# Reordering the head of the scan on ScalarE, VectorE and TensorE in a fused attention and expert kernel

## The chip, the cores and the metric

One core of a Trainium2 chip runs the whole program. The metric is the device time of one execution in microseconds (us). Three executions of the kernel before took 952.8, 953.1 and 955.27 us, median 953.1 us. Engines: PE is TensorE, DVE is VectorE, ACT is ScalarE, POOL is GpSimd, SP is SyncE, which issues most DMAs.

## What is computed

Three stages follow each other on 3072 tokens of width 384:

```python
# 1. delta rule attention, 32 heads of width 48, 768 steps
y[t] = q[t] @ state
state = state + beta[t] * outer(k[t], v[t] - k[t] @ state)      # k normalized
# 2. MLP 384 -> 2048 -> 384
h = x @ w_in;  g = maximum(0.01 * h, h);  x = g @ w_out
# 3. gated experts: argmax over 8 experts, two products 384 -> 1024 -> 384 for live tokens
y = gate_w * (maximum(x @ w1[e], 0) @ w2[e]);  out = x + y
```

## The kernel before, in words

The 768 steps are cut into G = 12 groups of 64. A group's recurrence is solved in closed form. It needs a product of k with the old state (z), the inverse of a small triangular system for each head (t, read as tT) applied to z (u), a correction (z2, u2), the output (y) and the new state (s). Each is done in two halves, r = 0 and r = 1. All matrices are fp16 pairs: a high half that ACT writes (a copy) and a low half, the rest after the high one, that DVE or POOL writes. Each product is three matmuls, high by high, low by high, high by low. So a scan step is a chain of PE product, DVE sum into fp32, ACT high half, DVE low half, next PE product.

The work is written out by hand as turns g with 16 steps f each; every engine has its own `turn` with the order of its steps. In a turn PE also runs the MLP: `up(g, f)` (L659 and on, first product, nine matmuls) and `down(g, f)` (L673 and on, second product, six matmuls), one of each in each step, shifted against the scan by 10 and 12 steps: in step f = 0 of turn g, `up` works on tile 6 of group g-1. Between them ACT does `hidden` (L937) and `hidden_high`, DVE `leaky` (L1294) and POOL `hidden_low` (L1604).

Other pieces that the change touches or that its steps meet:
- The head of the scan: PE `scan_z(g, r)` in f = 0, `scan_u(g, r)` in f = 1 (both L606, with s or z on the left). DVE `scan_z` (L1245) adds v to z, ACT `scan_z` writes its high half, DVE `scan_z_low` (L1250) its low half. `scan_u(g, 0)` on PE waits for that low half and for `t_loaded`.
- The inverse of group g+1 is made on DVE in 31 links (`inverse`, L1210 link 0, L1213 link 1, a wide product of 128x512, L1216 link 2, then pairs L1224 and L1230). `SHARE` says how many links a step takes, one half of them (rounded up) ahead of `leaky` and the rest behind. Links of group g+2 begin in f = 15. Link 0 waits for `seed`, an ACT copy of 128x1024 in f = 14. The finished inverse takes `inverse_high` (ACT, f = 12) and `inverse_low` (DVE, L1237, f = 12). Then SP writes it to DRAM with two DMAs (L443) and, when they have landed, reads it back with eight (L453): the landing of these is `t_loaded`.
- `q_low(g+2, x)` on DVE: low half of q, 64x768, in f = 13 and 15; the transposes of q by SP wait for it in the next turn.
- Rows and scores: ACT `rows_out(g-1)` in f = 11 copies the MLP's two accumulators b_acc (after `down` tile 15) to x2. `down` of the next group starts in them in f = 12. `gate_x` transposes x2 on PE, `gate_s` makes the scores on PE in f = 14 (w = 0) and f = 15 (w = 1), and DVE `gate_s` (L1303) copies them to `logit`. PE's second scores wait for DVE's first copy (same bank b_gr).
- `p_high(g+1, st)` on ACT in f = 11 to 14: high half of the masked q k products that DVE (L1186) has written.

L826 is the helper line of all ACT copies, L1157 that of DVE's low halves by `lo`.

Of the kernel before, what the change touches and what calls it, by code (L numbers as in the profile page):

```python
# [19 lines left out]
def build(nc, q, k, v, beta, w_in, w_out, w_skip, w_gate, w1, w2, out):  # L20
# [18 lines left out]
    TT = 2  # L39
# [19 lines left out]
    with ctx:  # L59
# [272 lines left out]
        def up_at(g, f):  # L332
            n = g if f >= 10 else g - 1
            return (n, (f - 10) % FT) if is_group(n) else None
# [19 lines left out]
        LINKS = 3 + 2 * (HR - 1)  # L354


        SHARE = (1, 1, 4, 0, 4, 2, 3, 1, 4, 3, 5, 4, 0, 0, 0, 1)

        SECOND = (2, 2, 2, 2, 3, 3, 2, 0, 0, 0, 6, 6, 5, 0, 0, 0)
        SOON = 14  # L360
# [206 lines left out]
        def _(pe):  # L567
# [104 lines left out]

            def down(g, f):  # L673
                pe.wait_ge(g_lo, FT * g + f + 1)
                if f == 0 and g:
                    pe.wait_ge(x2_ready, TT * g)
                elif f == 0:
                    pe.wait_ge(w_ready, DT + 4)
                for w in range(TT):
                    for a, b in PARTS:  # L680
                        mm = pe.matmul(b_acc[w][:, 0:DM], g16[:, f % 4, a, w * P:(w + 1) * P],  # L681
                                       wt[1][:, b, f * DM:(f + 1) * DM],
                                       start=(f == 0 and (a, b) == PARTS[0]),
                                       stop=(f == FT - 1 and (a, b) == PARTS[2]))
                mm.then_inc(acc_done, 1)
# [138 lines left out]
        def _(act):  # L824
# [80 lines left out]
            def scan_u(g, r):  # L905
                act.wait_ge(u_done, 2 * g + r + 1)
                copy(u16[:, HI, pair(r)], b_ch[r][:, 0:WR]).then_inc(u_hi, 1)
# [25 lines left out]
            def hidden(g, f):  # L933
                act.wait_ge(h_done, FT * g + f + 1)
                if FT * g + f >= 2:
                    act.wait_ge(g_ready, FT * g + f - 1)
                act.activation(r32[:, f % 2, :], b_h[f % 2][:, 0:GT], ACT.Relu, scale=0.99).then_inc(h_relu, 1)  # L937
# [7 lines left out]
            def rows_out(g):  # L945
                act.wait_ge(acc_done, FT * g + FT)
                if g:
                    act.wait_ge(x2_stored, 64 * g)
                    act.wait_ge(tr_done, tr_at["g", g - 1, TT - 1])
                for w in range(TT):  # L950
                    copy(x2[:, w, :], b_acc[w][:, 0:DM], 1.0 / (H_S * WO_S)).then_inc(x2_ready, 1)
# [38 lines left out]
            def turn(g):  # L990
                scan, nxt, ahead = is_group(g), is_group(g + 1), is_group(g + 2)
                gate, third = is_group(g - 1), is_group(g + 3)
                for f in range(FT):
                    if scan and f in (1, 3, 4, 6):
                        {1: scan_z, 3: scan_z2, 4: scan_u2, 6: scan_s}[f](g, 1)
                    if scan and f == 5:
                        scan_y(g, 1)
                    if gate and f in (13, 14):
                        gate_x(g - 1, f - 13)
                    if scan and f in (8, 9):  # L1000
                        x_high(g, f - 8)
                    if ahead and 7 <= f < 11:
                        gram_out(g + 2, f - 7)
                    if nxt and 11 <= f < 15:
                        p_high(g + 1, f - 11)
                    if nxt and f == (12 if g else 13):
                        inverse_high(g + 1)
                    if up_at(g, f):
                        hidden(*up_at(g, f))
                    if scan and f == 1:  # L1010
                        scan_u(g, 0)
                    if up_at(g, f):
                        hidden_high(*up_at(g, f))
                    if scan and f in (0, 2, 3, 4, 5):
                        {0: scan_z, 2: scan_z2, 3: scan_u2, 4: scan_y, 5: scan_s}[f](g, 0)
                    if g == G and f == 10:
                        act.wait_ge(h_done, FT * G)
                        split_hi(0, 0, 0)
                    if gate and f == 11:
                        rows_out(g - 1)  # L1020
                    if scan and f == 1:
                        scan_u(g, 1)
                    if nxt and f == 3:
                        a21_high(g + 1)
                    if g == 0 and f in (0, 1):
                        kn_high(2, f)
                    if third and f == k_part(g, "squares"):
                        squares(g + 3)
                    if third and f == k_part(g, "root"):
                        root(g + 3)  # L1030
                    if third and f - k_part(g, "split") in (0, 1):
                        kn_high(g + 3, f - k_part(g, "split"))
                    if ahead and f in (12, 13):
                        q_high(g + 2, f - 12)
                    if ahead and f == 14:
                        seed(g + 2)
                    if (g, f) in ((G - 1, 8), (G, 3)):
                        exponents(g - G + 1)
# [109 lines left out]
        def _(dve):  # L1148
# [174 lines left out]
            def turn(g):  # L1323
                scan, nxt, ahead = is_group(g), is_group(g + 1), is_group(g + 2)
                gate, third = is_group(g - 1), is_group(g + 3)
                sums = {0: scan_z, 2: scan_z2, 3: scan_u2, 5: scan_s}
                lows = {0: scan_z_low, 1: scan_u_low, 2: scan_z2_low, 3: scan_u2_low}
                for f in range(FT):
                    n, inv = (g + 2, ahead) if f >= SOON else (g + 1, nxt)
                    share = SECOND if n == 1 else SHARE  # L1330
                    at = sum(share[SOON:f]) if f >= SOON else sum(share[SOON:]) + sum(share[:f])
                    mid, end = at + (share[f] + 1) // 2, at + share[f]
                    if scan and f - 1 in sums:
                        sums[f - 1](g, 1)
                    if f == 0 and is_group(g - 2):
                        gate_s(g - 2, 1)
                    if f == 15 and gate:
                        gate_s(g - 1, 0)
                    if nxt and 11 <= f < 15:
                        gram_p(g + 1, f - 11)  # L1340
                    if inv and mid > at:
                        inverse(n, at, mid)
                    if gate and f in (13, 14):
                        gate_x_low(g - 1, f - 13)
                    if scan and f - 1 in lows:
                        lows[f - 1](g, 1)
                    if scan and f in (8, 9):
                        x_low(g, f - 8)
                    if up_at(g, f):
                        leaky(*up_at(g, f))  # L1350
                    if scan and f in sums:
                        sums[f](g, 0)
                    if inv and end > mid:
                        inverse(n, mid, end)
                    if scan and f in lows:
                        lows[f](g, 0)
                    if ahead and f in (13, 15):
                        q_low(g + 2, (f - 13) // 2)
                    if nxt and f == 4:
                        a21_low(g + 1)  # L1360
                    if nxt and f == (12 if g else 13):
                        inverse_low(g + 1)
                    if third and f == k_part(g, "sum"):
                        norm_sum(g + 3)
                    if third and f == k_part(g, "norm"):
                        norm(g + 3)
                    if g == G and f == 10:
                        split_lo(0, 0, 0)
                    if (g, f) in ((G - 1, 6), (G, 1)):
                        route_best(g - G + 1)  # L1370
                    if (g, f) in ((G - 1, 7), (G, 2)):
                        route_hot(g - G + 1)
                    if (g, f) in ((G - 1, 11), (G, 6)):
                        route_prob(g - G + 1)
                        route_rank(g - G + 1)
                    if g == G - 1 and f >= 12:
                        seats(2 * (f - 12), 2 * (f - 11))
                    if g == G and f < 9:
                        seats(2 * f + 8, min(2 * f + 10, NT - TT))
                    if g == 0 and f in (3, 4):  # L1380
                        split_w_out(f - 1)
                    if g == 0 and f in (4, 5):
                        q_low(1, f - 4)
# [372 lines left out]
```

## Time and profile before

| what | value |
|---|---|
| median of three executions | 953.1 us |
| the profiled execution | 950.53 us, its span 948.8 us |
| PE busy | 805.5 us, 85% |
| DVE busy | 644.0 us, 68% |
| ACT busy | 502.7 us, 53% |
| POOL busy | 412.1 us, 43% |
| mean granted PE clock | 0.944 |

The span begins with 130 us of loading and of a first, thinly filled turn. The turns run to about 705 us, the routing ends at about 720 us, and the experts take the rest. In the timeline a row has the start and the length in us, the engine, line and operation, what is written from what, and in brackets how long the engine had been idle before it and what ended that.

### The profile page before, as it was taken

What the parts mean: (1) busy time and instruction counts of PE and PEld (TensorE: products, weight loads), DVE (VectorE), ACT (ScalarE), POOL (GpSimd) and SP (SyncE); (2) the same over time, 40 slices, a digit from 0 to 9 for tenths busy, and PEclk for the clock granted to TensorE, in tenths of its full rate; (3) what the DMA queues carried; (4) which work ended last, traced back from release to release, by engine and by line L of the source; (5) the groups of instructions that cost most, each with busy time, mean ns of one, the idle gap of its engine ahead of it and who ended that gap; (6) DMA issues with size and microseconds to landing.
All of it is one profiled execution on the core that took longest, in us unless ns stands there. A gap on an engine that the chain in (4) does not pass through costs nothing.

```text
span 948.8 us, 27901 instructions
## 1 busy us (share of the span) xinstructions
PE 805.5 (85%) x10858; PEld 650.3 (69%) x10859; DVE 644.0 (68%) x1303; ACT 502.7 (53%) x1099; POOL 412.1 (43%) x500
## 2 busy tenths in 40 slices
PE   0314869899999999998989999999984899999986
PEld 0214648787777778787868777778753687788864
DVE  5478868787877778787877787765566835523372
ACT  4436546667575766566665657454453624322161
POOL 4404334536262635344453624253223655644463
PEclk9856699999999999999999999999995999999998
DMA  8774654575667766647656465332363943611100
GB/s 240 128 217 64 121 106 89 109 112 103 121 120 111 132 108 126 122 88 128 111 114 114 87 110 110 68 66 56 86 249 105 321 174 104 228 66 45 38 24 16
DMA packets 309830, 109.97 MB, mean 116 GB/s; under 512 B 284930, under 2 KB 301364, under 8 KB 309344
## 3 DMA queue, kind: packets, MB, share of 16 engines
q1 hardware_dynamic: 304000, 94.63, 48.0%
q0 software_dynamic: 3232, 7.64, 2.3%
q10 hardware_dynamic: 2496, 6.29, 1.8%
q8 instruction: 69, 1.13, 0.5%
q14 instruction: 33, 0.27, 0.1%
HBM read 60.39 MB, written 20.46 MB: 85 GB/s over the span
## 4 chain that ended last, share of the span: by engine, by line
PE 37%; DVE 24%; ACT 14%; issue 13%; DMA 6%; SPq 3%; POOL 2%; DVEq 1%; ACTq 0%; POOLq 0%
PE b_acc L807 8%; PE b_acc L681 8%; PE b_h L791 7%; PE b_h L668 7%; DVE stage L1294 5%; PE b_ch L606 4%; ACT ga L826 3%; ACT stage L937 3%; DVE inv L1230 2%; DVE inv L1224 2%; ACT stage L826 2%; ACT operands L826 2%; DMA natq<-x_dram,id_in 2%; ACT z L826 2%; DVE inv L1213 1%
## 5 line engine op out<-in xcount | busy, mean ns | idle before, releaser
L1604 POOL TENSOR_TENSOR stage<-stage 128x256 f16<-128x256 f32 x192 | 138.3, 720 | 289.5 <-ACT stage L826 288.6
L681 PE MATMUL b_acc<-wt,stage 128*128 128x384 f16 x1152 | 222.7, 331 | 6.2 <-ACT stage L826 5.7
L668 PE MATMUL b_h<-stage,wt 128*128 128x256 f16 x1728 | 221.7, 274 | 4.4 <-DVE stage L1294 3.2
L668 PEld LDWEIGHTS b_h<-stage,wt 128*128 128x128 f16 x1728 | 159.8, 98 | 24.6 <-DVE stage L1294 4.5
L681 PEld LDWEIGHTS b_acc<-wt,stage 128*128 128x128 f16 x1152 | 107.5, 98 | 63.2 <-POOL stage L1604 8.8
L826 ACT ACTIVATE stage<-stage 128x256 f16<-128x256 f32 x192 | 80.0, 417 | 125.5 <-DVE stage L1294 125.5
L1294 DVE SCALAR_TENSOR_TENSOR stage<-b_h,stage 128x256 f32<-128x256 f32 x192 | 80.9, 421 | 72.4 <-ACT stage L937 72.1
L807 PE MATMUL b_acc<-wt,operands 128*128 128x384 f16 x576 | 101.6, 327 | 6.0 <-DVE operands L1522 6.0
L791 PEld LDWEIGHTS b_h<-y,wt 128*128 128x128 f16 x1728 | 100.6, 100 | 8.3 <-issue 6.4
L791 PE MATMUL b_h<-y,wt 128*128 128x128 f16 x1728 | 103.3, 223 | 3.2 <-DVE y L1157 2.8
L572 PE MATMUL b_gr<-operands 128*128 128x128 f16 x576 | 45.1, 235 | 52.3 <-DMA operands<-operands 21.1
L1230 DVE TENSOR_REDUCE inv<-inv 128x30 f32<-128x90 f32 (+4 forms) x180 | 84.8, 471 | 5.6
L1594 POOL TENSOR_TENSOR operands<-masked,operands 128x512 f16<-128x512 f32 x48 | 57.2, 1193 | 70.1 <-ACT operands L826 70.0
L937 ACT ACTIVATE stage<-b_h 128x256 f32<-128x256 f32 x192 | 72.1, 375 | 22.5 <-PE b_h L668 22.5
L807 PEld LDWEIGHTS b_acc<-wt,operands 128*128 128x128 f16 x576 | 54.6, 98 | 39.5 <-DVE operands L1522 8.3
L572 PEld LDWEIGHTS b_gr<-operands 128*128 128x128 f16 x576 | 40.0, 106 | 57.0 <-issue 48.2
L1110 ACT ACTIVATE operands<-b_h 128x512 f16<-128x512 f32 x48 | 28.5, 594 | 85.1 <-PE b_h L791 85.1
L1224 DVE TENSOR_TENSOR inv<-a_sys,inv 128x60 f32<-128x60 f32 (+4 forms) x180 | 70.0, 389 | 1.8
L606 PE MATMUL b_ch<-z,operands 128*128 128x48 f16 x1152 | 40.2, 189 | 31.1 <-DVE z L1250 24.5
L606 PEld LDWEIGHTS b_ch<-z,operands 128*128 128x128 f16 x1152 | 38.1, 100 | 38.9 <-issue 29.7
L1522 DVE SCALAR_TENSOR_TENSOR operands<-b_h,operands 128x512 f16<-128x512 f32 x48 | 33.0, 688 | 46.1 <-ACT operands L1110 46.0
L1157 DVE SCALAR_TENSOR_TENSOR wt<-operands,wt 128x1536 f16<-128x1536 f32 x32 | 57.5, 1805 | 7.3 <-ACT wt L826 5.9
(174 smaller groups left out, 1300.9 us busy)
## 6 DMA issues: line engine op xcount, KB each, us to landing
operands<-in_moe_w_dram SPq DMA_DIRECT2D x16, 1536.0 KB, 7.0
a_sys<-a_dram SPq DMA_DIRECT2D x24, 256.0 KB, 4.2
natq<-in_q_dram SPq DMA_DIRECT2D x24, 192.0 KB, 4.0
raw_v<-in_v_dram SPq DMA_DIRECT2D x24, 192.0 KB, 3.7
stage<-y SPq DMA_DIRECT2D x96, 48.0 KB, 2.1
x_dram<-stage SPq DMA_DIRECT2D x24, 192.0 KB, 2.9
out_dram<-stage SPq DMA_DIRECT2D x24, 192.0 KB, 3.0
natk<-in_k_dram SPq DMA_DIRECT2D x22, 192.0 KB, 3.9
```

The lines of the kernel that those rows point to most:

```text
L572: mm = pe.matmul(b_gram[st % 2][:, p * P:(p + 1) * P], kT[g % 2][:, a, u, :], rhs[:, b, u, :], start=(p == 0 and (a, b) == PARTS[0]), stop ...
L606: mm = pe.matmul(b_ch[r][:, i * D:(i + 1) * D], lhs[:, a, u, :], rhs[:, b, u * D:(u + 1) * D], start=(first and i == 0 and (a, b) == PARTS ...
L668: mm = pe.matmul(b_h[f % 2][:, 0:GT], wt[0][:, a, d * FF + f * P:d * FF + (f + 1) * P], xT[:, g % 2, b, d, :], start=(i == 0), stop=(i == ...
L681: mm = pe.matmul(b_acc[w][:, 0:DM], g16[:, f % 4, a, w * P:(w + 1) * P], wt[1][:, b, f * DM:(f + 1) * DM], start=(f == 0 and (a, b) == PAR ...
L791: mm = pe.matmul(b_h[half][:, f * P:(f + 1) * P], wt[i][:, a, d * F1 + fc:d * F1 + fc + P], xgT[:, b, d * P:(d + 1) * P], start=(f == 0 an ...
L807: mm = pe.matmul(b_acc[0][:, 0:DM], e16[:, half, a, f * P:(f + 1) * P], wt[i][:, b, w0:w0 + DM], start=(half == 0 and f == 0 and (a, b) == ...
L826: return act.activation(o, i, ACT.Copy, scale=scale)
L937: act.activation(r32[:, f % 2, :], b_h[f % 2][:, 0:GT], ACT.Relu, scale=0.99).then_inc(h_relu, 1)
L1224: dve.tensor_tensor(inv[:, 1:3].rearrange("p k (r i) -> p k r i", i=BLK)[:, :, 0:rows, c:BLK], a[:, c - 2:c, c:BLK].unsqueeze(2).to_broadc ...
L1230: dve.tensor_reduce(t_next[:, 0:rows, c:BLK], planes.rearrange("p k (r i) -> p r i k", i=BLK)[:, 0:rows, c:BLK], AX.X, ALU.add).then_inc(t ...
L1294: dve.scalar_tensor_tensor(g32[:, f % 4, :], b_h[f % 2][:, 0:GT], 0.01, r32[:, f % 2, :], ALU.mult, ALU.add).then_inc(g_ready, 1)
L1604: pool.tensor_tensor(g16[:, f % 4, LO, :], g32[:, f % 4, :], g16[:, f % 4, HI, :], ALU.subtract).then_inc(g_lo, 1)
```

## The change

In `SHARE` (groups 2 and on) one link of the inverse moves from step 0 to step 1: link 1, the wide product, now stands in f = 1 ahead of `leaky`, and link 2 behind it. On DVE, `scan_z(g, 0)` moves to the front of step 0, ahead of the inverse and `leaky`; `q_low(g+2, 1)` moves to the front of step 15; the copy of the first scores moves from the front of step 15 to step 14. On ACT, `scan_z(g, 0)` moves between `hidden` and `hidden_high` of step 0; in step 11 `p_high(g+1, 0)` and `rows_out(g-1)` move between `hidden` and `hidden_high`. On PE, `down(g, 0)` waits for the two copies of x2 one at a time, each ahead of the matmuls that overwrite its accumulator. No instruction is added or removed.

```diff
--- before.py
+++ after.py
@@ -354,7 +354,7 @@
         LINKS = 3 + 2 * (HR - 1)
 
 
-        SHARE = (1, 1, 4, 0, 4, 2, 3, 1, 4, 3, 5, 4, 0, 0, 0, 1)
+        SHARE = (0, 2, 4, 0, 4, 2, 3, 1, 4, 3, 5, 4, 0, 0, 0, 1)
 
         SECOND = (2, 2, 2, 2, 3, 3, 2, 0, 0, 0, 6, 6, 5, 0, 0, 0)
         SOON = 14
@@ -672,11 +672,11 @@
 
             def down(g, f):
                 pe.wait_ge(g_lo, FT * g + f + 1)
-                if f == 0 and g:
-                    pe.wait_ge(x2_ready, TT * g)
-                elif f == 0:
+                if f == 0 and not g:
                     pe.wait_ge(w_ready, DT + 4)
                 for w in range(TT):
+                    if f == 0 and g:
+                        pe.wait_ge(x2_ready, TT * (g - 1) + w + 1)
                     for a, b in PARTS:
                         mm = pe.matmul(b_acc[w][:, 0:DM], g16[:, f % 4, a, w * P:(w + 1) * P],
                                        wt[1][:, b, f * DM:(f + 1) * DM],
@@ -1001,23 +1001,27 @@
                         x_high(g, f - 8)
                     if ahead and 7 <= f < 11:
                         gram_out(g + 2, f - 7)
-                    if nxt and 11 <= f < 15:
+                    if nxt and 12 <= f < 15:
                         p_high(g + 1, f - 11)
                     if nxt and f == (12 if g else 13):
                         inverse_high(g + 1)
                     if up_at(g, f):
                         hidden(*up_at(g, f))
+                    if nxt and f == 11:
+                        p_high(g + 1, 0)
+                    if scan and f == 0:
+                        scan_z(g, 0)
                     if scan and f == 1:
                         scan_u(g, 0)
+                    if gate and f == 11:
+                        rows_out(g - 1)
                     if up_at(g, f):
                         hidden_high(*up_at(g, f))
-                    if scan and f in (0, 2, 3, 4, 5):
-                        {0: scan_z, 2: scan_z2, 3: scan_u2, 4: scan_y, 5: scan_s}[f](g, 0)
+                    if scan and f in (2, 3, 4, 5):
+                        {2: scan_z2, 3: scan_u2, 4: scan_y, 5: scan_s}[f](g, 0)
                     if g == G and f == 10:
                         act.wait_ge(h_done, FT * G)
                         split_hi(0, 0, 0)
-                    if gate and f == 11:
-                        rows_out(g - 1)
                     if scan and f == 1:
                         scan_u(g, 1)
                     if nxt and f == 3:
@@ -1334,10 +1338,14 @@
                         sums[f - 1](g, 1)
                     if f == 0 and is_group(g - 2):
                         gate_s(g - 2, 1)
-                    if f == 15 and gate:
-                        gate_s(g - 1, 0)
+                    if ahead and f == 15:
+                        q_low(g + 2, 1)
+                    if scan and f == 0:
+                        scan_z(g, 0)
                     if nxt and 11 <= f < 15:
                         gram_p(g + 1, f - 11)
+                    if f == 14 and gate:
+                        gate_s(g - 1, 0)
                     if inv and mid > at:
                         inverse(n, at, mid)
                     if gate and f in (13, 14):
@@ -1348,14 +1356,14 @@
                         x_low(g, f - 8)
                     if up_at(g, f):
                         leaky(*up_at(g, f))
-                    if scan and f in sums:
+                    if scan and f in sums and f:
                         sums[f](g, 0)
                     if inv and end > mid:
                         inverse(n, mid, end)
                     if scan and f in lows:
                         lows[f](g, 0)
-                    if ahead and f in (13, 15):
-                        q_low(g + 2, (f - 13) // 2)
+                    if ahead and f == 13:
+                        q_low(g + 2, 0)
                     if nxt and f == 4:
                         a21_low(g + 1)
                     if nxt and f == (12 if g else 13):
```

## Rows read from the trace of the kernel before

**Rows 1.** The page: PE's granted clock in 40 slices, tenths of full speed

```profile
PEclk9856699999999999999999999999995999999998
```

**Rows 2.** Waits of PE over the span: us in total, times, longest

```profile
PE b_ch L606 <- DVE z L1250: 24.5, 11, 5.1
...
PE b_ch L606 <- DMA operands<-t_dram: 4.4, 2, 4.1
...
PE b_gr L708 <- DVE logit L1303: 2.0, 9, 0.2
```

**Rows 3.** Timeline of PE at the heads of turns 5 and 6

```profile
341.96 0.76 PE L606 MATMUL b_ch<-z,operands 128*128 128x48 f16 x24 [1.97 <-DVE z L1250]
...
387.19 0.77 PE L606 MATMUL b_ch<-s,operands 128*128 128x48 f16 x24
...
389.38 1.14 PE L668 MATMUL b_h<-stage,wt 128*128 128x256 f16 x9
392.48 0.71 PE L606 MATMUL b_ch<-z,operands 128*128 128x48 f16 x19 [1.96 <-DVE z L1250]
```

**Rows 4.** Timeline of DVE and ACT from turn 5's step 13 to turn 6's step 1

```profile
382.11 1.41 DVE L1157 SCALAR_TENSOR_TENSOR nq<-natq,nq 64x768 f16<-64x768 f32 x1
...
387.26 0.28 DVE L1210 SCALAR_TENSOR_TENSOR inv<-a_sys,inv 128x32 f32<-128x32 f32 x1 [1.42 <-issue]
387.47 0.42 DVE L1294 SCALAR_TENSOR_TENSOR stage<-b_h,stage 128x256 f32<-128x256 f32 x1
...
387.92 0.95 DVE L1157 SCALAR_TENSOR_TENSOR nq<-natq,nq 64x768 f16<-64x768 f32 x1
...
389.11 1.29 DVE L1213 TENSOR_TENSOR inv<-a_sys 128x512 f32<-128x512 f32 x1
...
390.65 0.54 DVE L1245 SCALAR_TENSOR_TENSOR scan<-raw_v,b_ch 128x384 f32<-128x384 f32 x1
...
391.22 0.52 ACT L826 ACTIVATE z<-scan 128x384 f16<-128x384 f32 x1
...
391.78 0.56 DVE L1250 TENSOR_TENSOR z<-scan,z 128x384 f16<-128x384 f32 x1 [0.59 <-ACT z L826]
...
392.73 0.68 DVE L1216 TENSOR_TENSOR a_sys<-a_sys,inv 128x512 f32<-128x512 f32 x1
```

**Rows 5.** Timeline: the inverse's low half in turns 5 and 6, SP's transfers of it

```profile
379.30 0.75 DVE L1237 TENSOR_TENSOR inv<-inv 128x256 f16<-128x256 f32 x2
...
431.29 0.75 DVE L1237 TENSOR_TENSOR inv<-inv 128x256 f16<-128x256 f32 x2
...
380.08 1.63 SPq L443 DMA_DIRECT2D t_dram<-inv  x2
383.48 5.32 SPq L453 DMA_DIRECT2D operands<-t_dram  x8
```

**Rows 6.** Timeline: the same low half and PE's product after it, turns 1 and 11

```profile
125.44 1.22 DVE L1237 TENSOR_TENSOR inv<-inv 128x256 f16<-128x256 f32 x2
...
137.13 0.58 PE L606 MATMUL b_ch<-z,operands 128*128 128x48 f16 x10 [4.10 <-DMA operands<-t_dram]
...
631.81 0.75 DVE L1237 TENSOR_TENSOR inv<-inv 128x256 f16<-128x256 f32 x2
...
643.54 0.78 PE L606 MATMUL b_ch<-z,operands 128*128 128x48 f16 x24 [0.31 <-DMA operands<-t_dram]
```

**Rows 7.** Timeline of turn 5, steps 11 and 12: rows, masked products, first down

```profile
376.20 0.85 ACT L826 ACTIVATE stage<-b_acc 128x384 f32<-128x384 f32 x2
...
377.38 0.63 ACT L826 ACTIVATE operands<-masked 128x512 f16<-128x512 f32 x1 [0.32 <-DVE masked L1186]
...
377.20 1.14 PE L681 MATMUL b_acc<-wt,stage 128*128 128x384 f16 x6 [0.69 <-ACT stage L826]
```

**Rows 8.** Windows at the head of turn 6: busy by engine, PE clock, DMA share

```profile
389.60:392.80 3.20, 1.24 (x22) 0.93 (x20) 2.61 (x6) 0.94 (x2) 0.67 (x1) 1.00 0.69 159
393.00:396.20 3.20, 3.20 (x41) 2.19 (x39) 2.14 (x6) 1.43 (x4) 0.67 (x1) 0.50 0.89 198
```

## The prediction

> **What bounds the kernel now.** I read the page first: PE is busy 85% of the span (table above), and its clock is full in nearly every slice from the sixth on [rows 1]. So a turn is set by PE's own work plus what PE waits for. The waits of PE name that: 24.5 us in 11 waits for the low half of z, 4.4 us for the inverse's transfer, 2.0 us for the copy of the first scores [rows 2]. The timeline shows where the first sits. In turn 6 PE starts `up` at 389.38, ends it at 390.52, and starts `scan_u(6,0)` only at 392.48 [rows 3]. The turn before had its own `scan_u(5,0)` at 341.96, so a turn takes 392.48 - 341.96 = 50.5 us.
>
> Why z is late stands on DVE [rows 4]. Link 0 waits 1.42 us; what releases it is the seed, a copy by ACT. Then come `leaky`, the second half of q (0.95), the scores copy, the wide product (1.29), `leaky` again (0.34 us to the start of the sum), and only at 390.65 the sum of z, though PE's z product had ended at 387.19 + 0.77 = 387.96 [rows 3]. After the sum come the ACT copy (0.52) and the low half, ended at 391.78 + 0.56 = 392.34.
>
> The second thing that `scan_u(g,0)` waits for is the inverse. Its low half ends at 379.30 + 0.75 = 380.05, SP issues two DMAs, then from 383.48 eight more, 5.32 us of issue [rows 5]. How long this trip takes to landing, two other heads tell, where PE did wait for it: 137.13 - (125.44 + 1.22) = 10.47 us in turn 1 and 643.54 - (631.81 + 0.75) = 10.98 us in turn 11 [rows 6]; mean 10.7. So in turn 6 it lands at about 380.05 + 10.7 = 390.8, and `scan_u` at 12.43 us after the low half is 1.7 us later than the inverse allows.
>
> **The clock.** In the window 389.6 to 392.8, where PE is busy 1.24 of 3.2 us, the granted clock is 1.00 (2.4 GHz); in the window behind it, 0.50 (1.2 GHz), with PE busy throughout [rows 8]. Heads 4, 8 and 10 have the same pair of windows, four falls in all. Its price: from `scan_u` to the inverse's next low half the turn after head 5 takes 380.05 - 341.96 = 38.09 us, the turn after head 6 takes 431.29 + 0.75 - 392.48 = 39.56 us [rows 3, 5], so 1.47 us a drop.
>
> **The change, part by part.**
>
> 1. Second half of q to the front of step 15. It now runs inside the 1.42 us in which DVE waits for the seed. It takes 0.95, or 1.41 as the first half does beside a POOL instruction [rows 4]; either end fits. Gain on DVE's chain ahead of z: 0.95. SP waits for it only in the next turn. Cost nothing, cover the seed.
>
> 2. Sum of z ahead of the inverse and `leaky`. With the wide product gone from step 0 too, DVE goes from link 0 (387.26) to `leaky` (0.21 later), 0.34 later to the scores copy, about 0.2 later to the sum: 388.0 on the old clock. The sum to the end of the low half took 392.34 - 390.65 = 1.69 [rows 4]. z would be ready at 389.7, 2.6 us earlier. `leaky(g-1,6)` moves behind the sum by 0.54, but DVE then waits 0.59 for ACT's z copy anyway, and this fills with it. `hidden_high` moves behind ACT's z copy (0.52); its `down` is a step and a half away.
>
> 3. The wide product in step 1. It stands between z's second sum and its second low half, where link 2 (half as long) stood. On my clock: sum 389.7 to 390.2, product to 391.5, low half to 392.0. PE asks for it 1.6 us after `scan_u(g,0)`: a scan product, a `down` and a scan product take 389.38 - 387.19 = 2.19 [rows 3], less the last, 0.6. With item 6 that is 392.0. Just hidden; link 2 falls behind `leaky`, ahead of u's low half, whose ACT copy is not out before. Cost 0, bound 0.6 a turn.
>
> 4. Step 11 on ACT, step 12 on PE. Now the rows copy stands behind `hidden_high`, which waits for `leaky`; it runs at 376.20 for 0.85, PE's `down` waits 0.69 for it until 377.20, and the masked copy (377.38) waits for DVE, which had `leaky` late because `hidden` was behind a waiting `p_high` [rows 7]. After: `hidden` first, so `leaky` need not wait its 0.4 us, and everything on DVE and ACT to the inverse's low half comes 0.4 us earlier. The rows copy is done before PE asks, so 0.69 goes on PE, and the separate waits for the two halves add nothing. `hidden_high` starts at most where it did.
>
> 5. First scores copy in step 14. PE's wait of 0.22 for it goes (2.0 in 9 turns) [rows 2]. DVE now waits for PE's scores in step 14; with PE 0.69 ahead by item 4 they are done first, and the ACT copy for the second rows had to wait for the same scores already, so nothing new is queued behind. Cost 0; if PE were not ahead, some 0.3 on `leaky`, which has that much slack.
>
> 6. Together. PE would be at `scan_u(6,0)` by 390.52 - 0.69 - 0.22 = 389.6, z is ready at 389.7 (389.3 with the 0.4 of item 4), but the inverse lands at 380.05 - 0.4 + 10.7 = 390.4. **The transfer becomes the bound.** A turn is then 38.1 - 0.4 + 10.7 = 48.4 us. PE's own part is 50.5 - 1.96 - 0.69 - 0.22 = 47.6, so PE still waits about 0.8 us at each head, now for t_dram.
>
> **The sum.** From head 1 to head 11 there are ten turns. Heads 2 to 10 each lose the 1.7 us by which `scan_u` came after the landing: 15.3. Ten low halves come 0.4 earlier: 4.2 (0.42 each, half of the 0.85 of the rows copy). The stall at a head falls from 1.96 to 0.8 us, so I take the four drops to go: 4 x 1.47 = 5.9. The loading, turn 0 (its head is bound by DVE's work, which stays the same) and the experts: 0. Total 25.4, and 0.2 for PE's short waits in turn 11: 25.6. The profiled execution took 950.5, so 924.9; the median of the runs stands 2.6 above it (953.1), so 927.5.
>
> **Rivals.**
>
> A. The transfer is faster or out of the way, and PE is the bound: all shown waits go, 2.87 a turn in nine turns, 25.8, and drops 5.9: 921.4. Against it: two measured trips of 10.5 and 11.0, made of issue time that the change doesn't touch. 8%.
>
> B. The drops stay, because the shorter waits still bring them. Then 5.9 is not gained: 933.4. For it: head 5 waited 1.97 us [rows 3] and had no fall, so the wait alone doesn't say when one comes. Against: every fall stands right behind such a wait, and the waits shrink. The Trainium skill (TensorE: Matmul & The Clock Gate, HAM oscillation) speaks against my reading: by its practical rule idle gaps as short as these don't bring the slow clock. By that rule the drops have another cause than the head's wait and stay, and the time is that of this rival. The trace has the fall right behind the wait in four heads and nowhere else between 150 and 700 us, so I follow the trace. 13%.
>
> C. The transfer's trip grows: SP's queue or the traffic beside it take 1 us more a turn, since transposes and loads keep their place while the turn shrinks. 10 us less gain: 937.5. 6%.
>
> D. Slower. The wide product sits on the chain. If the inverse lands so late that the first half gains nothing (trip above 12.4 us, which no row shows), only item 3 is left: z's second low half comes 0.6 us later (1.29 against 0.68 for link 2, which stood there [rows 4]), PE waits for it at `scan_u(g,1)`, 6 us in ten turns: 959. It decides where the second low half ends over 1.6 us after `scan_u(g,0)`. By my clock this is close (392.0 against 390.4 + 1.6), but a miss of tenths there only shaves the gain. 3%.
>
> That the change does nothing (z's sum moved but `leaky` or PE holding it as long) would give 953. z's product was ready long before the sum, so 1%.
>
> **How the numbers follow.** Forecast 69%, A 8, B 13, C 6, D 3, none 1. A measurement tells 0.3%, about 2.9 us, from no change here. All but D and the last are faster by much more: faster 0.95, same 0.02, slower 0.03. The range goes from A with a little more of the drop in turn 1 (919.5) to C (937.5); 924 to 931 is the forecast's own.
>
> **What would show it.** Right: in the waits of PE, "DVE z L1250" falls from 24.5 to the 5 of turn 0 and a little, and "DMA operands<-t_dram" rises from 4.4 to over 10; head to head 48.4 us in the middle; clock 1.00 from 150 to 700; L1213 between two L1245 and L1250; q's second half where DVE idled 1.42; PE's `down` in step 12 without a wait. Wrong: PE waits at `scan_u(g,1)` or at `leaky` (L1294) in step 0, a slow window at the heads, or t_dram landing more than 11 us after L1237.

## The result and the profile after

The kernel after takes 931.91 us (median of four, 930.35 to 934.12) against 954.18 us before (median of four on the same chip). The ratio is 0.9775, 95% interval 0.9753 to 0.9796: faster by 2.25%, some 22 us, where 25.6 were forecast (927.5 against 953.1). The profiled execution after took 934.12 us, span 932.4.

The page after, first line and granted clock, as [rows 1]:

```profile
span 932.4 us, 27901 instructions
...
PEclk9975698999999999999999999999986999999998
```

Below, head k is the start of PE's first u product of turn k, and the turn to head k runs from head k-1 to head k. Two windows of the same trace, from just ahead of head 1 (139.3) to behind turn 11 (columns as in [rows 8]):

```profile
137.00:145.00 8.00, 5.70 (x68) 4.22 (x69) 2.07 (x5) 1.28 (x3) 0.67 (x1) 0.57 0.99 189
145.00:690.00 545.00, 532.63 (x7645) 431.99 (x7642) 429.66 (x964) 348.45 (x854) 241.60 (x277) 1.00 0.59 113
```

The same stretch before, with PE busy 527.43 of 555 us:

```profile
145.00:700.00 555.00, 527.43 (x7528) 426.82 (x7525) 416.67 (x950) 342.86 (x840) 235.44 (x273) 0.99 0.58 110
```

So PE is busy 97.7% of the middle in place of 95.0%, at full clock (2.4 GHz) from 145 us on: the four falls behind heads 4, 6, 8 and 10 are gone.

PE's waits after, against [rows 2]:

```profile
PE b_ch L606 <- DMA operands<-t_dram: 10.8, 9, 4.5
...
PE b_ch L606 <- DVE z L1254: 6.8, 2, 6.3
...
PE b_acc L681 <- POOL stage L1612: 0.4, 2, 0.2
```

The wait for z is that of turn 0 (6.3 of the 6.8); at the later heads PE waits for the inverse's transfer alone. The wait for the scores copy and that for the rows copy are not there any more.

PE at the heads of turns 4 and 5, against [rows 3]:

```profile
285.58 1.14 PE L668 MATMUL b_h<-stage,wt 128*128 128x256 f16 x9
287.49 0.78 PE L606 MATMUL b_ch<-z,operands 128*128 128x48 f16 x24 [0.76 <-DMA operands<-t_dram]
...
334.48 1.14 PE L668 MATMUL b_h<-stage,wt 128*128 128x256 f16 x9
336.04 0.78 PE L606 MATMUL b_ch<-z,operands 128*128 128x48 f16 x24 [0.42 <-DMA operands<-t_dram]
```

This turn takes 336.04 - 287.49 = 48.55 us where it took 50.5. The seven turns to heads 3 to 9 take 48.6 to 49.7, mean 49.0. At heads 2 to 9 PE waits 0.2 to 1.6 us for t_dram (1.6 at head 6); at heads 10 and 11 it doesn't.

DVE at the head of turn 5, against [rows 4]:

```profile
331.01 1.29 DVE L1161 SCALAR_TENSOR_TENSOR nq<-natq,nq 64x768 f16<-64x768 f32 x1
332.47 0.43 DVE L1214 SCALAR_TENSOR_TENSOR inv<-a_sys,inv 128x32 f32<-128x32 f32 x1 [0.18 <-issue]
332.82 0.41 DVE L1298 SCALAR_TENSOR_TENSOR stage<-b_h,stage 128x256 f32<-128x256 f32 x1
333.16 0.15 DVE L1307 TENSOR_SCALAR logit<-b_gr 128x9 f32<-128x9 f32 x1
333.23 0.54 DVE L1249 SCALAR_TENSOR_TENSOR scan<-raw_v,b_ch 128x384 f32<-128x384 f32 x1
...
334.40 0.56 DVE L1254 TENSOR_TENSOR z<-scan,z 128x384 f16<-128x384 f32 x1
334.88 0.55 DVE L1249 SCALAR_TENSOR_TENSOR scan<-raw_v,b_ch 128x384 f32<-128x384 f32 x1
335.34 1.26 DVE L1217 TENSOR_TENSOR inv<-a_sys 128x512 f32<-128x512 f32 x1
336.51 0.55 DVE L1254 TENSOR_TENSOR z<-scan,z 128x384 f16<-128x384 f32 x1
```

q's second half fills the wait for the seed (idle 0.18 in place of 1.42). The low half of z ends at 334.96, 1.1 us ahead of the product that uses it (0.5 to 2.3 at heads 2 to 11). The wide product stands between z's second sum and second low half, and this ends at 337.06, 0.6 us ahead of its product (336.04 + 1.6).

The inverse's low half and SP's transfers, against [rows 5]:

```profile
324.77 0.75 DVE L1241 TENSOR_TENSOR inv<-inv 128x256 f16<-128x256 f32 x2
...
325.55 1.12 SPq L443 DMA_DIRECT2D t_dram<-inv  x2
328.65 5.66 SPq L453 DMA_DIRECT2D operands<-t_dram  x8
```

From the low half's end (325.52) to PE's release is 10.5 us; this is the trip. From the head before to the low half it is 325.52 - 287.49 = 38.03 us; before it was 38.09. **This is the step that did not come true**: 0.4 us less was forecast. The cause shows in step 11 of the same turn (DVE, ACT, POOL, PE; against [rows 7]):

```profile
320.39 0.41 DVE L1298 SCALAR_TENSOR_TENSOR stage<-b_h,stage 128x256 f32<-128x256 f32 x1
320.49 0.85 ACT L826 ACTIVATE stage<-b_acc 128x384 f32<-128x384 f32 x2
320.66 1.16 POOL L1602 TENSOR_TENSOR operands<-masked,operands 128x512 f16<-128x512 f32 x1 [0.78 <-ACT operands L826]
320.73 1.17 DVE L1228 TENSOR_TENSOR inv<-a_sys,inv 128x60 f32<-128x60 f32 x1
...
321.93 0.28 DVE L1234 TENSOR_REDUCE inv<-inv 128x30 f32<-128x90 f32 x1
...
321.85 1.14 PE L681 MATMUL b_acc<-wt,stage 128*128 128x384 f16 x6
```

The same two instructions before, in turn 5:

```profile
375.19 1.16 POOL L1594 TENSOR_TENSOR operands<-masked,operands 128x512 f16<-128x512 f32 x1 [0.79 <-ACT operands L826]
...
375.76 0.67 DVE L1224 TENSOR_TENSOR inv<-a_sys,inv 128x60 f32<-128x60 f32 x1
```

and after, in turn 9, where POOL's instruction begins behind the product:

```profile
564.80 0.21 DVE L1228 TENSOR_TENSOR inv<-a_sys,inv 128x60 f32<-128x60 f32 x1
565.03 1.16 POOL L1602 TENSOR_TENSOR operands<-masked,operands 128x512 f16<-128x512 f32 x1 [1.52 <-ACT operands L826]
```

`leaky` does end earlier (0.57 us against the head before) and PE's `down` does start without a wait. But the next DVE instruction, a product of 128x60, takes 1.17 us beside POOL's low half of p and ends with it; before, it began 0.56 us later beside the same POOL instruction, took 0.67 and ended at the same place of the turn. This is so in each of the turns 1 to 8 of both traces (1.16 to 1.18 us and 0.66 to 0.67). With no POOL instruction beside it the product takes 0.21. So what was won ahead of it went into waiting. The kernel after shows the other case too: in turns 9 and 10 the product runs ahead of POOL's instruction, and there the low half does come earlier, by 0.3 us (36.19 against 36.45) and by some 0.4 us (34.05 against 35.92, of which 1.47 is the price of a fall).

Where the time went, head 1 to head 11 (ten turns), worked out of both traces:

```
                                             before   after    gain
head g to the inverse's low half, ten sums   382.8    376.8     6.0
low half to landing, ten sums                107.0    108.4    -1.5
landing to PE's product, ten sums             16.7      0.6    16.1
sum                                          506.4    485.8    20.6
```

The first line holds the four falls (5.9 at 1.47 each; 39.5 against 38.0 us behind heads 4, 6 and 8), 1.1 us of earlier low halves (0.05 to 0.07 behind each of heads 2 to 8, the rest behind heads 9 and 10), and 1.0 lost behind head 1, where the slow clock lasted longer. The other stretches of this execution were slower than in the profiled one before: up to head 1 by 2.2 us, behind head 11 by 2.0, which is why the spans differ by 16.4 only while the medians differ by 22. These two stretches scatter by as much in the traces of all the kernels here (136.6 to 139.6 and 305.3 to 307.6 us).

### The profile page after: what moved, and what is told of

Its sections match the earlier page's. It is cut to its first block, busy times and chain, and to the rows that moved or that the text cites. A ratio compares the mean times of both kernels' runs of the same rounds, so it can differ in the third digit from the quotient of the medians.

```text
span 932.4 us, 27901 instructions
## 1 busy us (share of the span) xinstructions
PE 801.2 (86%) x10858; PEld 648.3 (70%) x10859; DVE 650.3 (70%) x1303; ACT 500.6 (54%) x1099; POOL 415.9 (45%) x500
## 4 chain that ended last, share of the span: by engine, by line
PE 61%; DMA 11%; DVE 9%; SPq 7%; issue 4%; ACT 4%; POOL 3%; DVEq 0%; POOLq 0%; ACTq 0%
PE b_acc L681 16%; PE b_h L668 15%; PE b_ch L606 9%; PE b_acc L807 8%; PE b_h L791 7%; SPq L453 4%; DMA natq<-x_dram,id_in 3%; PE b_gr L572 3%; DMA operands<-t_dram 3%; DMA t_dram<-inv 3%; PE b_ch L572 2%; DMA natq<-in_q_dram 1%; DVE inv L1234 1%; ACT inv L826 1%; DVE inv L1228 1%
## 5 line engine op out<-in xcount | busy, mean ns | idle before, releaser
L1612 POOL TENSOR_TENSOR stage<-stage 128x256 f16<-128x256 f32 x192 | 142.4, 742 | 266.7 <-ACT stage L826 266.0
L681 PE MATMUL b_acc<-wt,stage 128*128 128x384 f16 x1152 | 219.4, 327 | 2.4 <-POOL stage L1612 0.4
L826 ACT ACTIVATE stage<-stage 128x256 f16<-128x256 f32 x192 | 80.0, 416 | 98.7 <-DVE stage L1298 97.7
L572 PE MATMUL b_gr<-operands 128*128 128x128 f16 x576 | 44.6, 233 | 53.1 <-DMA operands<-operands 20.6
L1228 DVE TENSOR_TENSOR inv<-a_sys,inv 128x60 f32<-128x60 f32 (+4 forms) x180 | 74.9, 416 | 1.8
L606 PE MATMUL b_ch<-u,operands 128*128 128x48 f16 x1728 | 56.9, 186 | 0.3 <-DVE u L1259 0.3
L606 PEld LDWEIGHTS b_ch<-u,operands 128*128 128x128 f16 x1728 | 53.9, 98 | 3.8 <-issue 0.4
```

The costliest lines, as they stand in the source:

```text
L572: mm = pe.matmul(b_gram[st % 2][:, p * P:(p + 1) * P], kT[g % 2][:, a, u, :], rhs[:, b, u, :], start=(p == 0 and (a, b) == PARTS[0]), stop ...
L606: mm = pe.matmul(b_ch[r][:, i * D:(i + 1) * D], lhs[:, a, u, :], rhs[:, b, u * D:(u + 1) * D], start=(first and i == 0 and (a, b) == PARTS ...
L826: return act.activation(o, i, ACT.Copy, scale=scale)
L1228: dve.tensor_tensor(inv[:, 1:3].rearrange("p k (r i) -> p k r i", i=BLK)[:, :, 0:rows, c:BLK], a[:, c - 2:c, c:BLK].unsqueeze(2).to_broadc ...
L1612: pool.tensor_tensor(g16[:, f % 4, LO, :], g32[:, f % 4, :], g16[:, f % 4, HI, :], ALU.subtract).then_inc(g_lo, 1)
```

## The experiments

All are edits of the kernel after, except where it says before. Ratios are to the kernel before, run on the same chip; they carry the comparisons, since not all experiments ran on one chip. The middle is the time from head 1 to head 11 of the profiled execution (506.4 us before, 485.8 after). Diffs are cut to the lines that matter.

### One half alone, then the other

`e1_head_only`: step 11's order, the split wait and the early scores copy undone.

```diff
-                if f == 0 and not g:
+                if f == 0 and g:
+                    pe.wait_ge(x2_ready, TT * g)
+                elif f == 0:
...
-                    if f == 0 and g:
-                        pe.wait_ge(x2_ready, TT * (g - 1) + w + 1)
...
-                    if nxt and 12 <= f < 15:
+                    if nxt and 11 <= f < 15:
...
+                    if f == 15 and gate:
+                        gate_s(g - 1, 0)
```

> The kernel after with its step 11 order on ScalarE, its split wait on TensorE and its early first scores copy undone: only the head of the scan is changed. Theory (the inverse's transfer sets the turn): TensorE's own part of a turn rises by the 0.69 and 0.22 us of those two waits to about 48.5, still under the 48.9 of scan_u to inverse ready (38.0) plus trip (10.9). So the time is that of the kernel after, 932, within 2 us, and TensorE's waits for t_dram shrink by some 0.7 us a head. Rival (each part brings its own share): 0.9 us a turn are lost, 8 to 9 us, so 940.

Measured: 933.63 us, ratio 0.9769 (0.9729 to 0.9809). PE's waits, 130 to 650 us:

```profile
PE b_ch L606 <- DMA operands<-t_dram: 9.7, 8, 3.7
PE b_acc L681 <- ACT stage L826: 5.3, 8, 0.7
PE b_gr L708 <- DVE logit L1305: 1.9, 9, 0.2
```

The two small waits are back, up to 0.7 and 0.2 us each time, and cost nothing that can be measured: PE would otherwise wait longer for the transfer. (The middle was 488.9 us against 485.8, and 1.9 of these 3.1 us are longer trips.)

`e2_rows_only`: the other half alone, the head as before.

```diff
-        SHARE = (0, 2, 4, 0, 4, 2, 3, 1, 4, 3, 5, 4, 0, 0, 0, 1)
+        SHARE = (1, 1, 4, 0, 4, 2, 3, 1, 4, 3, 5, 4, 0, 0, 0, 1)
...
-                    if scan and f == 0:
-                        scan_z(g, 0)
```

> The other half alone: step 11, split wait and early scores copy as in the kernel after, the head of the scan as before. Theory: the chain of VectorE to the low half of z sets the head as before and the 0.69 us that TensorE wins in step 12 go into a longer wait for z; so 950 to 954, falls of the clock at the heads remain or grow. Rival: parts add, 944.

Measured: 953.82 us, ratio 0.9997 (0.9978 to 1.0015). The page's clock and PE's waits, 130 to 650 us:

```profile
PEclk9965799999999999999999999999995999999998
```

```profile
PE b_ch L606 <- DVE z L1252: 21.2, 9, 2.6
PE b_ch L606 <- DMA operands<-t_dram: 4.3, 2, 4.1
```

Nothing is gained. The wait for z grew to 2.3 us, 2.6 at one head, and the granted clock fell behind seven heads in place of four, each time for 3.4 us. A turn without a fall took 50.2 us, 0.3 less than before (50.5); over the turns this small gain is taken back by the three falls more (4.4 us). So the whole gain of the change belongs to the head. That the longer wait brings more falls fits; no experiment here sets when a fall comes, so this one run doesn't prove it.

### The order at the head

`e4_share_back`: the wide product in step 0 again, behind the sum of z.

```diff
-        SHARE = (0, 2, 4, 0, 4, 2, 3, 1, 4, 3, 5, 4, 0, 0, 0, 1)
+        SHARE = (1, 1, 4, 0, 4, 2, 3, 1, 4, 3, 5, 4, 0, 0, 0, 1)
```

> The kernel after with the wide product back in step 0 (ahead of leaky but behind the sum of z). Theory: z's first low half comes 0.7 to 1.3 us later, of which 0.9 to 1.8 us a head were hidden behind the transfer: 932 to 934. Rival (the wide product on the way of z matters as it did before): 1.3 us in each of ten turns, 945.

Measured: 934.95 us, ratio 0.9800 (0.9763 to 0.9837). The middle took 486.6 us, 0.8 more than in the kernel after; the low half of z comes 0.9 us later and still ahead of the transfer in seven full turns. The place of the wide product is worth little as long as the transfer is the bound.

`e8_q_low_back`: q's second low half behind `leaky` again.

```diff
-                    if ahead and f == 15:
-                        q_low(g + 2, 1)
...
-                    if ahead and f == 13:
-                        q_low(g + 2, 0)
+                    if ahead and f in (13, 15):
+                        q_low(g + 2, (f - 13) // 2)
```

> The kernel after with q's second low half back behind leaky in step 15. Theory: link 0 then waits idle for the seed and z's low half comes 0.95 us later; the heads had 0.9 to 2.2 us to spare against the transfer, so most of it is hidden: 932 to 934, with TensorE waiting for z in some heads again. Rival (q's place carries a share of its own): 0.95 in each of nine turns, 940.

Measured: 937.01 us, ratio 0.9823 (0.9794 to 0.9851), between the theory and the rival. PE's waits, 130 to 650 us:

```profile
PE b_ch L606 <- DMA operands<-t_dram: 13.8, 8, 4.5
PE b_ch L606 <- DVE z L1254: 2.3, 5, 0.8
```

z is late in five products, up to 0.8 us. Behind heads 2, 3, 4 and 8, where its second low half is late or just in time, it is 38.2 to 38.4 us to the inverse's low half where it was 38.0 (1.8 us over ten turns). The trips took 1.3 us more, and from landing to PE's product it was 1.0 more; together these make the 4.2 us that the middle is longer (490.0). The theory of pure cover was too simple here: with 0.95 us less, the margin is used up in part of the turns. By the medians, of the two pieces of the head undone alone this one cost more; the intervals of e4 and e8 overlap.

### Why the low half came no earlier

`e3_pair_moved`: one product and one sum of the inverse in step 9 in place of step 11, so that no link stands beside POOL's low half of p.

```diff
-        SHARE = (0, 2, 4, 0, 4, 2, 3, 1, 4, 3, 5, 4, 0, 0, 0, 1)
+        SHARE = (0, 2, 4, 0, 4, 2, 3, 1, 4, 5, 5, 2, 0, 0, 0, 1)
```

> The kernel after with two links of the inverse moved from step 11 to step 9, so that no link is left beside GpSimd's low half of p. Theory (the 0.4 us that step 11 should have given were taken back by the product of the last pair of links, which took 1.17 us in place of 0.67 and ended with GpSimd's instruction beside it): the inverse is ready 0.4 us or more earlier in each turn, 37.6 after scan_u in place of 38.0, and ten turns give 4 us: 928. Rival (the order on ScalarE sets it): 38.0 stays, 932.

Measured: 934.18 us, ratio 0.9776 (0.9737 to 0.9815). The low half is ready 37.3 us after the head in place of 38.0, as the theory says and more (the product of 128x60 now runs ahead of `leaky`, in 0.26 us; 0.2 of the 0.7 can be its own length, which left the way). Yet the time stays: over ten turns the low halves gain 5.8 us and the trips lose 7.3. SP's queue in one turn, the read of a_sys, the inverse's write and its read:

```profile
322.30 1.57 SPq L436 DMA_DIRECT2D a_sys<-a_dram  x2
324.12 1.12 SPq L443 DMA_DIRECT2D t_dram<-inv  x2
328.28 6.29 SPq L453 DMA_DIRECT2D operands<-t_dram  x8
```

and in the kernel after:

```profile
322.81 1.54 SPq L436 DMA_DIRECT2D a_sys<-a_dram  x2
```

The write is now issued 0.3 us after the read of a_sys has been issued, where 1.2 us lay between (in most other turns 1.3 where it was 2.7). For heads 2 to 8 it lands 3.4 to 4.8 us after the low half, where the shortest take 2.9 (in the kernel after five of these seven land after 2.9 to 3.1). The trip to heads 3 to 8 is 11.3 to 12.7 us in place of 10.5 to 11.7. PE's waits show a second price, 0.75 us in nine turns for the low half of x, ahead of which more of the inverse now stands:

```profile
PE b_ch L606 <- DMA operands<-t_dram: 9.9, 6, 4.4
PE b_h L668 <- DVE stage L1161: 6.8, 9, 0.8
```

`e7_pair_k_load_behind`: the same, with the load of k moved on SP's queue.

```diff
-                if is_group(g + 4):
-                    load_k(g + 4)
...
                 if is_group(g - 1):
                     x2_out(g - 1)
+                if is_group(g + 4):
+                    load_k(g + 4)
```

> Two links moved from step 11 to step 9 as in e3, and the load of k of the fourth group ahead moved on SyncE's queue from ahead of the read of the small systems (a_sys) to behind the rows. Theory (in e3 the inverse was ready 0.7 us earlier, but its write then ran beside the read of a_sys and landed 3.4 to 4.8 us after the low half in place of 2.9): with the load of k away the read of a_sys is over sooner, the write lands after 2.9 to 3.5, the trip is back near 11, a turn takes 48.2: 926 to 929. Rival (the trip ends at a time of its own whatever is done): 933.

Measured: 931.35 us, ratio 0.9768 (0.9736 to 0.9800). The mechanism came (the write lands after 2.9 to 3.5 us in all turns but one, the trip is 10.1 to 11.5; the middle is 484.1), the time did not: in most turns PE reaches the head after the landing, because it waits for the low half of x. The waits, 130 to 650 us:

```profile
PE b_h L668 <- DVE stage L1161: 7.8, 10, 1.0
PE b_ch L606 <- DMA operands<-t_dram: 5.1, 4, 4.4
```

`e10_k_load_behind`: only the load of k moved, on the kernel after.

> The kernel after with only the load of k behind the rows on SyncE's queue. Theory (k's load, 192 KB issued 3 to 5 us ahead of the inverse's write, is what makes the trip vary between 10.3 and 11.7): the trip is 10.4 to 10.8 throughout, 0.3 us less a turn, 3 us: 929. Rival (the variation comes from the transfers behind, or is noise): 932.

Measured: 932.06 us, ratio 0.9774 (0.9747 to 0.9802). Trips of 10.0 to 11.7 us, as in the kernel after. The diff is the one of e7. The rival holds: that load is not what makes them vary. What does is open.

### A shorter trip

`e5_four_reads_after`: four reads in place of eight; the layout in DRAM is changed so that the two halves of a block of 32 rows lie side by side.

```diff
-        t_w = t_dram.rearrange("h q u l r i -> h (q u) (l r i)")
...
+        t_w = t_dram.rearrange("q u l r h i -> h (q u) (l r) i")
...
                 for b in range(4):
-                    for h in range(2):
-                        sp.dma_start(tT[BLK * b + h:BLK * b + BLK:2, :, :, BLK * b:BLK * b + BLK].rearrange(
-                            "r u l i -> r (u l) i"), t_r[h, b]).then_inc(t_loaded, 16)
+                    sp.dma_start(tT[BLK * b:BLK * b + BLK, :, :, BLK * b:BLK * b + BLK].rearrange(
+                        "p u l i -> p (u l) i"), t_r[b]).then_inc(t_loaded, 16)
```

> The kernel after with the inverse read back from DRAM by four DMAs in place of eight (its layout in DRAM is changed for that, so the two writes go in pieces of 64 bytes). Theory (the transfer sets the turn): the issue of the read is some 2.7 us shorter, the write perhaps 1 us longer; the trip falls from 10.8 to 8.5 to 9.5. Then z's low half, 0.9 to 2 us ahead of scan_u until now, is the bound, a turn takes some 47.8 us and the time is 920 to 925. Rival (TensorE or the order on VectorE sets the turn by now, the trip only happens to end there): 932 stays.

Measured: 927.88 us, ratio 0.9728 (0.9700 to 0.9756), the middle 481.2 us. The write lands after 4.8 to 5.9 us (it took 2.9: more than the 1 us I allowed), the trip is 9.4 to 10.8 us. PE's waits, 130 to 650 us:

```profile
PE b_ch L605 <- DMA operands<-t_dram: 5.8, 6, 3.6
PE b_h L667 <- DVE stage L1297: 1.5, 1, 1.5
```

The transfer is the bound of the kernel after, or nothing would have come of this. At the heads at which it lands early (6, 7, 10 and 11) PE doesn't wait, and z is ready 0.5 us before: PE's own queue is the last. The turns to heads 6 and 7 take 48.0 and 48.2 us, of which PE is busy 47.6 and 47.8.

`e6_four_reads_before`: the same edit in the kernel before.

> The same shorter read in the kernel before. Theory: there the transfer lands 1.4 to 2.4 us ahead of scan_u in the turns 2 to 10, so a shorter one gives nothing in these; heads 1 and 11 gain 1 to 2 us: 951 to 954. Rival (the transfer is a bound of its own in both kernels): 10 us or more gained, 943.

Measured: 953.2 us, ratio 0.9991 (0.9974 to 1.0008). The same edit is worth nothing where z is late, and 4 us where it isn't (927.88 against 931.91; by the ratios 4.5).

`e9_four_reads_pair_k_load`: e5 and e7 together.

> The three together on the kernel after: four reads in place of eight, two links moved to step 9, the load of k behind. In e5 and e7 the heads with a trip under 10 us had TensorE itself as the bound, at 48.0 to 48.6 us a turn. Theory: with the inverse ready at 37.4 and a trip of 10.2 TensorE is the bound in all turns, at 48.1; against e5's mean of 48.4 in turns 3 to 9 this gives 2 to 3 us: 925 to 927. Rival (still the transfer): another 0.7 us a turn as in t_ready, 921.

Measured: 928.79 us, ratio 0.9739 (0.9714 to 0.9764), no better than e5. PE is the bound in nine of ten turns, but at 48.5 us; its waits in the middle:

```profile
PE b_h L667 <- DVE stage L1160: 7.8, 10, 1.0
PE b_ch L605 <- DMA operands<-t_dram: 4.1, 2, 3.5
```

More of the inverse in step 9 stands ahead of the low half of x. This is the second price that e3 and e7 showed, and the expectation had left it out: PE's turn is longer by that wait.

`e11_four_reads_pair_step10`: e5 with the links in step 10.

```diff
-        SHARE = (0, 2, 4, 0, 4, 2, 3, 1, 4, 3, 5, 4, 0, 0, 0, 1)
+        SHARE = (0, 2, 4, 0, 4, 2, 3, 1, 4, 3, 7, 2, 0, 0, 0, 1)
```

> Four reads as in e5, and two links moved from step 11 to step 10 in place of step 9. Theory (in e9 the links in step 9 stood ahead of the second low half of x, and TensorE waited 0.75 us a turn for it): that wait is gone, the inverse is still ready before 37.7, TensorE is bound at 48.0 to 48.1 a turn: 925 to 926. Rival (more links in step 10 hold leaky, or the write meets the read of a_sys as in e3): 928 to 930.

Measured: 926.48 us, ratio 0.9704 (0.9684 to 0.9724), the best of all: some 6.8 us (0.9775 less 0.9704, of 954) under the kernel after, 1.4 us under e5 by the medians, which is inside the spread. PE's waits:

```profile
PE b_ch L605 <- DMA operands<-t_dram: 7.8, 7, 3.4
PE b_h L667 <- DVE stage L1160: 1.2, 2, 1.0
```

The wait for x is nearly gone, the low half is ready after 37.4 us, the turns to heads 4 to 9 take 47.4 to 48.7. The trip grew again to 9.9 to 11.1, so that the transfer is the bound of most turns once more.

## Why the prediction was right, and where it was off

The mechanism was right in each part that decides. z's low half was forecast 2.6 to 3.0 us earlier against the turn; it came 2.9 earlier (47.5 us behind the head before in place of 50.4) and stopped being the last. The transfer was forecast as the next bound: t_dram is PE's releaser at heads 1 to 9. The size of a turn was off: 48.4 us were forecast, the turns to heads 3, 4, 5 and 7 took 48.55 to 48.87, and those to heads 6, 8 and 9 took 49.3 to 49.7. So the median of 931.9 us lies 4.4 above the forecast, 0.9 outside the narrow range of 924 to 931 and closer to rival B's 933.4; it is the trace, in which the falls are gone, that tells the two apart. By the steps:

- Items 1 to 3 (head): as forecast. e1 and e2 show that the gain is here, and e8 that the place of q carries more than its cover suggests. Item 3's wide product is just hidden: z's second low half ends 0.3 to 1.8 us ahead of its product at heads 2 to 9, and 0.15 ahead at head 10, which is how close it stands where PE did wait for z.
- Item 4 (step 11): this step failed in part. `leaky` and ACT's masked copy were to carry 0.4 us on to the inverse's low half; DVE's next product waited them away beside POOL. Ten turns at 0.42 made 4.2 us of the forecast; 0.06 came in a full turn and 1.1 us in all. e3 shows that without that product there the low half does come earlier, by 0.7, and e11 by 0.6. The working had the rows of both instructions but added the time as if the length of the DVE product were its own.
- The waits of 0.69 and 0.22 on PE went, and e1 shows them worth nothing, as item 6 says: PE was not the bound.
- The trip, 10.7 from two heads: mean 10.84 at heads 2 to 11 after, 10.70 at the same heads before. Off by 0.1 to 0.2 a turn, 1.5 us in all. Single trips reached 11.65, and each counts now that nothing covers it. Trips of over 11 us were one of the prediction's own signs of being wrong; they came at heads 1, 6, 8 and 9 (11.1 to 11.65), and why they vary is open.
- The slack of 1.7 a head: 15.3 forecast, 16.1 gained.
- The falls of the clock: 5.9 forecast, four falls gone, 5.9. The price of 1.47 a fall was right. Heads 2 to 11 of the kernel after had none, with waits of 0 to 1.6 us, nor had those of the nine experiments that keep the sum of z in front, with waits up to 1.9. Of nine heads with waits of 1.96 to 2.2 us four had one in the kernel before and five in e6; of nine with 2.3 to 2.6 us in e2, seven. The rival by the Trainium skill (TensorE: Matmul & The Clock Gate, HAM oscillation), that so short gaps don't bring the slow clock, did not hold in this kernel: idle times of 1.96 to 2.6 us were often followed by it. Rival B is out.
- Head 1, where z is no help and PE waits for t_dram: the window from 137 to 145 us stood at 0.57 in place of 0.80 before, 1 us lost. This is not the change's doing as far as the runs show: the slow stretch there lasts 3.4 us in some traces (before, e2, e3, e4, e5, e9) and 6.8 in the others, e6 with the head as before among them.
- Rival A (PE's own bound) was put at 47.6 us a turn. PE is busy 47.6 of a turn; e5 shows turns of 48.0 and 48.2, since `up` in step 0 waits 0.1 for `leaky` and two `down` wait 0.26 together for POOL. With two links moved (e11) these waits shrink and a turn without a wait at its head took 47.4. Rivals C and D did not come, though e3 showed C's mechanism: the write met the read of a_sys.

In sum the middle gave 20.6 us where 25.4 stood. Of the 4.8 that are missing 3.1 are item 4, 1.5 the trip and 1.0 the slow clock at head 1, against 0.8 more from the slack.

## What to carry to other kernels

Before moving the step that an engine waits for, find the landing or end of everything else that it waits for: here the transfer landed only 1.7 us ahead of z, and that set the gain. Time won on a chain is kept only if the next instruction's length is its own: look at what runs beside it on GpSimd, and at what the transfer behind it will meet. Small waits on an engine that is not the bound were worth nothing here (0.91 us a turn in e1), whatever they add up to.

## What was unexpected

A VectorE product of 128x60 that takes 0.21 us alone took 0.67 or 1.17 us beside a GpSimd instruction of 1.16 us and ended within 0.1 us of it in both cases, so that its start made no difference. And waits of TensorE of 2 us were followed by a fall to 1.2 GHz of 3.4 us, worth 1.47 us each, in about half of the heads, and waits of 2.3 us and more in seven of nine. So in four turns taking away the wait of about 2 us paid 1.47 us more than the time waited.
